# A fused delta-rule attention and two expert layers on one core: the first corner product handed over in two parts, and filler products moved and added

## The reference, cut to what matters

```python
# q, k, v: (4, 8, 768, 48); beta: (4, 8, 768)
k_n = k / (norm(k) + 1e-6)
for t in range(S):
    y[:, :, t] = q_t @ state
    v_old = state . kn_t
    state = state + beta_t * outer(kn_t, v_t - v_old)
x = y as (3072, 384)
h = max(max(x @ w1, x @ w2), x @ w3)          # 384 -> 768
x = h @ w_out                                 # 768 -> 384
# third layer: 8 experts, the two best per token by noisy gates,
# out += gate * (relu(x @ w1[e]) @ w2[e])     # 384 -> 1024 -> 384
```

## Time and profile before

| | us |
|---|---|
| median of three timed runs | 1019.89 (1019.06 to 1021.56) |
| the profiled execution | 1013.34 |
| its span, first to last instruction | 1011.3 |
| TensorE matmul busy | 992.2 (98%) |
| DVE busy | 727.0 (72%) |
| ACT busy | 465.4 (46%) |
| POOL busy | 219.8 (22%) |
| mean granted TensorE clock | 0.986 of full |

### The profile page before, as it was taken

How to read it: one execution, slowest core, us unless ns; L and a number is a source line. 1 busy time by engine, 2 the same in 40 slices (tenths; PEclk the granted TensorE clock), 3 DMA queues, 4 the chain that set the end, 5 groups by cost and what they waited for, 6 DMA issues and landing times.

```text
span 1011.3 us, 26066 instructions
## 1 busy us (share of the span) xinstructions
PE 992.2 (98%) x10597; PEld 923.1 (91%) x10597; DVE 727.0 (72%) x1701; ACT 465.4 (46%) x694; POOL 219.8 (22%) x235
## 2 busy tenths in 40 slices
PE   8999999999999999999999999999999999999995
PEld 7788898898898898898899999999999999999995
DVE  6978796886895885435578767767777677776872
ACT  4553245235225325223455556545565465655551
POOL 0484300220210220222134122121221212212111
PEclk8799999999999999999999999999999999999998
DMA  9450320510420330235765534253352616525121
GB/s 327 98 126 2 96 53 24 154 38 24 131 63 3 86 86 3 70 113 180 246 206 130 158 57 159 46 147 73 47 167 55 164 38 172 177 60 154 38 29 23
DMA packets 71191, 101.70 MB, mean 101 GB/s; under 512 B 28608, under 2 KB 59584, under 8 KB 70720
## 3 DMA queue, kind: packets, MB, share of 16 engines
q1 hardware_dynamic: 59024, 78.10, 25.3%
q0 software_dynamic: 10992, 20.70, 10.8%
q10 hardware_dynamic: 1088, 1.65, 0.5%
HBM read 136.98 MB, written 29.51 MB: 165 GB/s over the span
## 4 chain that ended last, share of the span: by engine, by line
PE 94%; DVE 4%; ACT 1%; issue 0%; POOLq 0%; POOL 0%; DVEq 0%; ACTq 0%
PE ps L2002 46%; PE ps L2165 20%; PE ps L2050 8%; PE ps L1808 4%; PE ps L2176 3%; PE ps L1932 2%; PE ps L1960 2%; PE ps L1789 2%; PE ps L1949 2%; PE ps L2066 2%; PE ps L1901 1%; PE ps L1866 1%; DVE prod L1234 1%; DVE x L1238 1%; PE ps L1912 1%; PE ps L2152 1%
## 5 line engine op out<-in xcount | busy, mean ns | idle before, releaser
L2002 PE MATMUL ps<-xr,wr_in 128*128 128x512 f32 x972 | 234.0, 396 | 0.3 <-ACT xr L944 0.3
L2002 PEld LDWEIGHTS ps<-xr,wr_in 128*128 128x128 f32 x972 | 179.3, 188 | 39.2 <-issue 0.3
L2002 PE MATMUL ps<-xbT,w1r 128*128 128x256 f32 x1728 | 211.6, 284 | 0.6
L2002 PEld LDWEIGHTS ps<-xbT,w1r 128*128 128x128 f32 x1728 | 209.7, 192 | 2.5 <-issue 2.1
L2165 PE MATMUL ps<-w2r,hbT 128*128 128x384 f32 x1152 | 205.9, 336 | 0.0
L2165 PEld LDWEIGHTS ps<-w2r,hbT 128*128 128x128 f32 x1152 | 198.9, 188 | 0.0
L779 POOL DMA_INDIRECT out_rows<-yb,idx x55 | 90.6, 1647 | 374.1 <-DVE yb L1590 288.4
L1021 ACT ACTIVATE hbT<-ps 128x512 fp32r<-128x512 f32 x96 | 57.3, 597 | 166.1 <-PE ps L2002 166.1
L1402 DVE TENSOR_TENSOR w1r<-w1s,w1r 128x768 fp32r<-128x768 f32 x124 | 117.4, 956 | 17.2 <-ACT w1r L1005 15.1
L1005 ACT CAST w1r<-w1s 128x768 fp32r<-128x768 f32 x124 | 101.2, 827 | 24.9 <-DMA w1s<-in_we 24.9
L1402 DVE TENSOR_TENSOR w2r<-w2s,w2r 128x768 fp32r<-128x768 f32 x124 | 110.2, 951 | 1.5 <-ACT w2r L1009 1.5
(11 more groups left out here) (247 smaller groups left out, 1132.4 us busy)
## 6 DMA issues: line engine op xcount, KB each, us to landing
w1s<-in_we SPq DMA_DIRECT2D x31, 1536.0 KB
w2s<-in_we SPq DMA_DIRECT2D x31, 1536.0 KB
xb<-rows SPq DMA_DIRECT2D x24, 402.0 KB, 4.0
kv_s<-in_kv SPq DMA_DIRECT2D x24, 384.0 KB, 3.4
k_s<-in_k SPq DMA_DIRECT2D x12, 512.0 KB, 3.9
joint<-in_q SPq DMA_DIRECT2D x24, 256.0 KB, 4.8
out_rows<-padrow SPq DMA_DIRECT2D x13, 384.0 KB, 4.7
w_in<-in_w_blocks SPq DMA_DIRECT2D x3, 1152.0 KB, 11.4
```

What stands on the lines that cost most here:

```text
L2002: mm = pe.matmul(dst, w, m, start=(opens and n == 0), stop=(closes and n == len(todo) - 1))
```

## The change

On ACT and DVE the corner of the first chunk is copied in two instructions of half the size instead of one, each behind its own semaphore (`corner_half(0)` and `corner_half(1)`); `first_corner(0)` signals after each half of its 32 products; `solve_u(0)` waits for the first half of the corner ahead of its first 16 products, and for the second ahead of the other 16. Of the fillers, eight products of 128 columns and 23 of 32 by 32 now stand behind `gram(1)`; the four wide ones in `blocks_to_rows` become four short ones each; the last wide one goes; and 13 of 32 by 32 stand in the first tile behind its fifth `h_product`. The `corner_half` shown is ACT's; DVE's is the same for rows 64 to 95 with a multiplication by -1, and the second list entry that the diff shows (`first_corner_half`) is DVE's.

```diff
+            def corner_half(n):
+                act.wait_ge(p_corner_first if n else p_corner_half, 1)
+                act.wait_ge(s_solve_first, 1)
+                h_, g = half_places(n)[n]
                 nc.scalar.activation(
-                    by_bank_pair(solve[0:Q, n * PAIRS:(n + 1) * PAIRS, Q:L]),
-                    ps[0:Q, first_banks(n):first_banks(n) + 2, 0:HP * Q].rearrange("p g (a t) -> p g a t", t=Q), ACT.Copy,
-                    scale=-1.0).then_inc(s_corner if n else s_corner_first, 1)
+                    solve[0:Q, g * HP:(g + 1) * HP, Q:L],
+                    ps[0:Q, first_banks(0) + g, 0:HP * Q].rearrange("p (a t) -> p a t", t=Q), ACT.Copy,
+                    scale=-1.0).then_inc(s_corner_first if n else s_corner_half, 1)
...
-            first_corner(0)
+            corner_half(0)
+            corner_half(1)
...
-            first_corner_half(0)
+            corner_half(0)
+            corner_half(1)
...
+            def small_fillers(bank, n):
+                for _ in range(n):
+                    pe.matmul(ps[0:Q, bank, 0:Q], ones[0:Q, 0:Q], ones[0:Q, 0:Q], start=True, stop=True)
...
                     if i % 8 == 7:
-                        keep_warm_wide(C_BANKS)
+                        keep_warm(C_BANKS, 4)
...
-                turns(one).then_inc(p_corner if n else p_corner_first, 1)
+                if n == 0:
+                    half_turns(one, 0).then_inc(p_corner_half, 1)
+                    half_turns(one, 1).then_inc(p_corner_first, 1)
+                else:
+                    turns(one).then_inc(p_corner, 1)
...
-                    pe.wait_ge(s_corner_first, 2)
+                    pe.wait_ge(s_corner_half, 2)
...
+                elif c == 0:
+                    half_turns(one, 0)
+                    pe.wait_ge(s_corner_first, 2)
+                    half_turns(one, 1).then_inc(p_u, 1)
...
             gram(1)
+            keep_warm(C_BANKS, 8)
+            small_fillers(C_BANKS, 23)
             gram(2)
...
             keep_warm(C_BANKS, 2, Q - 2)
-            keep_warm_wide(C_BANKS)
...
                         out_product(t, i - PRODUCTS)
+                    if t == 0 and i == 4:
+                        small_fillers(E_BANKS + 1, 13)
```

More of the change, by code:

```diff
@@ L232, in build @@
         s_corner = sem("corner_ready")
+        p_corner_half = sem("first_chunk_corner_half_in_psum")
+        s_corner_half = sem("first_chunk_corner_half_ready")
         s_corner_first = sem("first_chunk_corner_ready")
@@ L840, in first_solve, with second_corner @@
                                          scale=high_rows[:, 0:1]).then_inc(s_solve if n else s_solve_first, 1)
-            def first_corner(n):
-                act.wait_ge(p_corner if n else p_corner_first, 1)
-                act.wait_ge(s_solve if n else s_solve_first, 1)
+            def corner_half(n):
+                act.wait_ge(p_corner_first if n else p_corner_half, 1)
+                act.wait_ge(s_solve_first, 1)
+                h_, g = half_places(n)[n]
                 nc.scalar.activation(
-                    by_bank_pair(solve[0:Q, n * PAIRS:(n + 1) * PAIRS, Q:L]),
-                    ps[0:Q, first_banks(n):first_banks(n) + 2, 0:HP * Q].rearrange("p g (a t) -> p g a t", t=Q), ACT.Copy,
-                    scale=-1.0).then_inc(s_corner if n else s_corner_first, 1)
+                    solve[0:Q, g * HP:(g + 1) * HP, Q:L],
+                    ps[0:Q, first_banks(0) + g, 0:HP * Q].rearrange("p (a t) -> p a t", t=Q), ACT.Copy,
+                    scale=-1.0).then_inc(s_corner_first if n else s_corner_half, 1)
+            def second_corner():
+                act.wait_ge(p_corner, 1)
+                act.wait_ge(s_solve, 1)
+                nc.scalar.activation(
+                    by_bank_pair(solve[0:Q, PAIRS:2 * PAIRS, Q:L]),
+                    ps[0:Q, first_banks(1):first_banks(1) + 2, 0:HP * Q].rearrange("p g (a t) -> p g a t", t=Q), ACT.Copy,
+                    scale=-1.0).then_inc(s_corner, 1)
             def first_state():
@@ L1060, in _ @@
             u_out(0)
[L1061 removed]
+            second_corner()
             first_state()
@@ L1300, in diagonals_of, with corner_half, second_corner @@
                 last.then_inc(s_diag, 1)
-            def first_corner_half(n):
-                dve.wait_ge(p_corner if n else p_corner_first, 1)
-                dve.wait_ge(s_solve if n else s_solve_first, 1)
+            def corner_half(n):
+                dve.wait_ge(p_corner_first if n else p_corner_half, 1)
+                dve.wait_ge(s_solve_first, 1)
+                h_, g = half_places(n)[1 - n]
                 rows = slice(L, L + Q)
                 nc.vector.tensor_scalar(
-                    by_bank_pair(solve[rows, n * PAIRS:(n + 1) * PAIRS, Q:L]),
-                    ps[rows, first_banks(n):first_banks(n) + 2, 0:HP * Q].rearrange("p g (a t) -> p g a t", t=Q), -1.0, None,
-                    ALU.mult).then_inc(s_corner if n else s_corner_first, 1)
+                    solve[rows, g * HP:(g + 1) * HP, Q:L],
+                    ps[rows, first_banks(0) + g, 0:HP * Q].rearrange("p (a t) -> p a t", t=Q), -1.0, None,
+                    ALU.mult).then_inc(s_corner_first if n else s_corner_half, 1)
+            def second_corner():
+                dve.wait_ge(p_corner, 1)
+                dve.wait_ge(s_solve, 1)
+                rows = slice(L, L + Q)
+                nc.vector.tensor_scalar(
+                    by_bank_pair(solve[rows, PAIRS:2 * PAIRS, Q:L]),
+                    ps[rows, first_banks(1):first_banks(1) + 2, 0:HP * Q].rearrange("p g (a t) -> p g a t", t=Q), -1.0, None,
+                    ALU.mult).then_inc(s_corner, 1)
             def first_state():
```

2 lines of the change are left out of this document (1 added, 1 removed).

## The result

| us | before | after |
|---|---|---|
| median of 22 timed runs each, taken side by side | 1019.95 (1018.07 to 1023.06) | 1022.39 (1019.1 to 1026.72) |
| the profiled execution | 1013.34 | 1022.15 |
| its span | 1011.3 | 1020.0 |
| mean granted TensorE clock | 0.986 | 0.984 |

What follows compares the result with a forecast made beforehand. It took TensorE as the bound from 65.24 us, and before that DVE's inversion to 37.4, then TensorE. +0.9 (clock on the path, split included) and +1.0 (first tile) made +1.9 on 1019.89: 1021.8, range 1016.5 to 1024.5.

Steps and rivals of the forecast that it cites:

- the likeliest class: Whole kernel: time within 0.3% of no change, neither below 1016.8 nor above 1023.0 us; chance 0.70.
- Corner in two parts, -0.25: Before solve_u(0): DVE's first half copy takes about 0.43 us instead of 0.70, so solve_u(0) starts 0.25 us earlier.
- Fillers behind gram(1): In the start: 1.9 plus 1.4 us of fillers cost nothing, give gram(2) and gram(3) full clock, fold 3.9 us.
- The gain of 1.7 us for k times q: Behind the fold, which ends at 20.9 instead of 22.64 us: k times q and the blocks move up 1.7 us.
- It is idle for 2.3 us: After the second pair's blocks end at 34.7 us: TensorE idles 2.3 us, works 0.5, idles 1.9 more.
- I expect the clock to fall at 37 to 41 us: Before or in the low products: half clock slows the path through solve_u(0) to the state step, +0.9 us.
- Fillers in the first tile: Behind the fifth h_product: 13 small products take 0.8 us plus 0.2 for interrupting, paid in full, +1.0 us.
- dear fillers: Rival, first tile: small fillers cost 0.12 us a pass like wide ones, +4.2 in all, 1024.1 us; chance 0.10.
- no overlap: Rival, first tile: passes at one place don't overlap, 26 take 7.8 us, time 1028.8; chance 0.03.
- The clock holds: Rival, solve: full clock throughout, or back before solve_u; -1.5 us in all, 1018.4; chance 0.17.
- The clock falls where it does now: Rival, solve: half clock from 44.4 to 51.2 us as before; +0.7 us in all, 1020.6; chance 0.20.
- Hidden half clock: Rival, timed runs: their extra 6.55 us is partly half clock, the change removes some 4 us, 1016; chance 0.08.

Runs made afterwards that it cites:

- e1: Only the corner split in two parts, all fillers as in the kernel before; median 1020.36 against 1020.02, ratio 1.0004.
- e11: The changed kernel run again, unaltered, against the kernel before on a third chip; median 1015.71 against 1013.74, ratio 1.002.
- e6: The kernel before with only the 8 and 23 fillers behind gram(1) added; median 1023.9 against 1019.13, ratio 1.0043.
- e10: The changed kernel with 18 small fillers moved from behind gram(1) to the first tile; against the kernel before, 1016.31 to 1013.74, ratio 1.0024.
- e0: The kernel before, unchanged, run for a second trace; median 1020.39 against 1020.02, ratio 1.0004.
- e7: The kernel before with only the fillers among the second pair's blocks changed; median 1021.57 against 1019.13, ratio 1.0014.
- e2: The changed kernel without the 13 fillers of the first tile; against the kernel before, median 1026.97 to 1020.02, ratio 1.0071.
- e8: The changed kernel with the load of w_o delayed until the blocks are done; against the kernel before, median 1020.07 to 1014.29, ratio 1.0057.
- e3: The kernel before with only the 13 small fillers in the first tile added; median 1020.86 against 1020.02, ratio 1.0013.
- e4: The kernel before with 42 small fillers added in the first tile; median 1026.66 against 1019.13, ratio 1.0064.
- e5: The kernel before with 64 small fillers added in the first tile; median 1026.11 against 1019.13, ratio 1.0059.
- e9: The kernel before with only the corner split and the load of w_o delayed until the blocks are done; median 1014.11 against 1014.29, ratio 0.9993.

## Why the prediction was right, and where it was right for the wrong reason

The time came out within 0.6 us and in the likeliest class, but a step that carries half of the sum failed, so the closeness is in part luck. Term by term:

- **Corner in two parts, -0.25**: right. DVE's half took 0.43 us, as reckoned from the copies of the earlier trace rows; the first alone releases solve_u(0), and the middle wait is absent. e1 shows 0.57 us of idleness for 0.87.
- **Fillers behind gram(1)**: they took 1.64 us for the 46 small passes (1.4 forecast) and 2.05 for the 16 large (1.9), and gram(2) and gram(3) got full clock. Wrong is the fold: I took 3.9 us at full clock, and in after and e11 the clock fell within it (6.12 and 5.91 us), as it had at 20.49 in before, a fall that I left out of my reading. In e6, e10, e0 and e7 it took 4.19. The gain of 1.7 us for k times q didn't come in after (24.01, with 23.90 in before). It came in e6 and e10 (21.55 and 21.70), but e0 and e7, without a filler behind gram(1), have 21.95 and 21.92. The means over all traces are 22.88 with these fillers and 23.43 without, a difference of 0.6 us, where two executions of the same kernel (before and e0) are 1.95 apart.
- **"It is idle for 2.3 us", and "I expect the clock to fall at 37 to 41 us", +0.9**: this step failed. The blocks ended at 39.02 and not at 34.7, late by the fold, the half clock up to 35.60 and the standstill, so TensorE was never idle from 30.3 to 42.7, and the clock was full from 35.60 on. It fell at 45.90, less than 1 us into the solve as before, and for as long. None of the six traces with changed fillers among the blocks (after, e2, e7, e8, e10, e11) had the two idle stretches. The most there was before the low product is 0.49 us, in e10. In the place of this term stands a later solve, by 1.75 us, and a first h_product later by 1.83, behind 1.80 us of standstill and the longer half clock in the blocks. That 1.80 and 1.75 lie so close doesn't make the one the cause of the whole other: the 3.1 us by which the blocks were late hold both. The size depends on the pair of executions too: after is 0.90 later than e0, e11 1.45 later than before and 0.52 later than e0. By the prediction's own statement, that 0.50 from 37 to 41 would show it, the step is wrong, and the sum was right since a loss that I didn't know of has about the same size: 2.4 us measured less 1.2 for the first tile leaves some 1.2, where I had 0.9.
- **Fillers in the first tile, +1.0**: right in size, 1.17 in after and 1.15 in e3. But "nothing hides it" was only half of the story. In the company of the others the 13 fillers are worth about -4.7 us (e2 against after), by their number and not their work: e4 and e5 show that the shift does it. In the traces 2.9 of these can be seen, less 1.2 of their own; the other 3 us lie between the medians and are not placed. The median of e2 rests on five runs.
- **Of the rivals**, *dear fillers* and *no overlap* are refuted by the 0.93 us for 26 passes. The Trainium skill ("TensorE: Matmul & The Clock Gate", Part 3, The mechanism) says of the weight load that it overlaps a running matmul only where the row group differs; 26 passes in one row group, of 0.108 of load and 0.191 of matmul, in 0.93 us, don't agree with that, and the measurement decides. *The clock holds* didn't come in any trace of after; full clock through the solve came in e5 and e9, with the first h_product at 64.98 and 63.90. *The clock falls where it does now* is what happened, but not at the price that I had given it (+0.7), for want of the standstills. *Hidden half clock*: the 6.55 us turned out to be of another kind, since e0 has the time and a granted clock of 0.987, with 0.986 in the first trace.

What stays open: why the transfer of a block begins late in one execution and not in the next. In five of the 20 (e0, the second of e6, e7, the second of e8, the first of e10) it began within 0.4 us of when TensorE stopped, or after it (e7: stopped at 33.25, transfer 33.45 to 34.95, on at 36.46), and these are five of the six that are over 2.4 us. In all five the kernel's own loads were just running out: the DMA share fell from 1.41 to 0.74 in e0, from 1.18 to 0.50 in e6, from 1.43 to 0.47 in e7, from 1.38 to 0.46 in e10 and from 1.07 to 0.05 in e8, each from one half microsecond to another 1 us later, 1.5 in e7. So a block that queues behind the loads is still a live rival for the large ones. Against it, other blocks came through amid loads (in before from 28.29 to 29.52), and the standstills of the tiles, up to 1.03 us, have hardly a load beside them (DMA shares of 0.00 to 0.02 in e2). Why the clock fell in the fold of after and e11 but not in e10 is open too. That TensorE waits for the block is inferred from the number, from the one transfer for each 256 instructions and from the nearly constant distance to the landing; no run takes the loading away. And each kernel has one trace, so what a stretch costs is known for single executions alone. Nor did any version beat both kernels; the best, e9, is level with before (0.9993).

## What to carry to other kernels

Before reading two traces against each other, run the unchanged kernel once more on the same chip: here 5.6 of the 8.7 us between the traces were there without the change. An instruction that does no work has two prices, its own time and the shift of everything behind it in the program; where a variant with less work is slower, count TensorE's instructions up to each "issue" gap. And a filler that keeps the clock must be paid for by a stretch on the critical path that gains from it; these stood where DVE's inversion set the time anyway.

## What the runs showed of the hardware

- TensorE can stand still for 0.46 to 3.21 us with nothing to wait for that the profile shows, where the count of its instructions reaches 192 or 193 above a multiple of 256 inside a dense run of small products (20 times in 14 traces), and goes on 1.27 to 1.75 us after a 16.4 kB block of instructions has landed. Between the large products of the h_products (512 columns, 0.230 us each) there was none over 0.15.
- A 32 by 32 fp32 pass repeated at one place of the array takes 36 ns (46 in 1.64 us, 26 in 0.93, both at full clock), twice the 16 ns of passes that alternate between two places.
- The clock can fall though TensorE is busy without a break: in the fold of before at 20.49 and of after at 18.57, and behind 42 and 64 small fillers in e4 and e5. The Trainium skill ("TensorE: Matmul & The Clock Gate", What's actually happening) calls the slow state the default that activity releases; here the profile has TensorE busy for all of the 3.60 us before it fell in e5.
- The same program was about 6 us faster on one chip than on two others (medians of 1013.7 to 1014.3 and of 1019.1 to 1020.0). On the slower two the traces have idle moments of 0.12 to 0.41 us at fixed places of the tiles, 2.8 us of the 5.6 in e0; on the faster one there are none at these places.
